# First-layer weights of an attention + MoE kernel split once and kept in DRAM, instead of split again in every quarter

## What is computed

```python
scores = scale * np.matmul(q, k.transpose(0, 1, 3, 2))
kth = np.partition(scores, -32, axis=-1)[..., -32:-31]
scores = np.where(scores >= kth, scores, -1000000000.0)
attn = softmax(scores)            # exp(s - max) / (sum + 1e-9)
x = heads_to_columns(attn @ v)    # 1152 x 512
h = x @ w_in                      # 512 x 2048
x2 = (h * (1.0 / (1.0 + np.exp(-h)))) @ w_out
P = balanced(exp(x2 @ w_gate))    # 1152 x 8
for e in range(8):
    out += P[:, e:e + 1] * (np.maximum(x2 @ w1[e], 0.0) @ w2[e])   # w1: 512 x 1024
```

## Time and profile before

| | |
|---|---|
| median of 3 runs | 1369.2 us (1368.82 to 1369.33) |
| the profiled execution: span from first to last instruction | 1366.2 us |
| between that span and the median | 3.0 us |
| first quarter (attention alone) | to about 118 us |
| quarters with attention and slices | about 118 to 507 us |
| slices alone | about 507 to 562 us |
| experts | from about 562 us |
| TensorE busy | 1350.0 us, 99% |
| VectorE, ScalarE, GpSimd busy | 733.3, 490.3, 351.1 us |
| DMA | 82.16 MB in packets, 18.5% of the engines' time |

### The profile page before, as it was taken

How to read it: one execution, slowest core, us unless ns; L and a number is a source line. 1 busy time by engine, 2 the same in 40 slices (tenths; PEclk the granted TensorE clock), 3 DMA queues, 4 the chain that set the end, 5 groups by cost and what they waited for, 6 DMA issues and landing times.

```text
span 1366.2 us, 21083 instructions
## 1 busy us (share of the span) xinstructions
PE 1350.0 (99%) x8021; PEld 1197.5 (88%) x8021; DVE 733.3 (54%) x1561; ACT 490.3 (36%) x1040; POOL 351.1 (26%) x305
## 2 busy tenths in 40 slices
PE   8999999999999999999999999999999999999999
PEld 6887888788878889989989989989989988998997
DVE  6999989998999975652222222222222222222222
ACT  3446766766675645402112202202211211211210
POOL 0004434534553543212112202202202211211200
PEclk9999999999999999999999999999999999999999
DMA  2033223222231223211011001001101101101001
GB/s 55 23 95 110 89 66 114 84 84 86 90 119 54 93 94 124 93 63 62 19 44 62 31 31 61 31 30 61 61 0 61 61 0 61 61 17 45 0 0 69
DMA packets 59745, 82.16 MB, mean 60 GB/s; under 512 B 17568, under 2 KB 25760, under 8 KB 59680
## 3 DMA queue, kind: packets, MB, share of 16 engines
q1 hardware_dynamic: 59680, 81.30, 18.5%
HBM read 78.92 MB, written 2.36 MB: 59 GB/s over the span
## 4 chain that ended last, share of the span: by engine, by line
PE 94%; DVE 3%; DMA 1%; ACT 1%; issue 1%; POOL 0%; SPq 0%; ACTq 0%
PE banks L322 24%; PE banks L323 24%; PE banks L324 23%; PE banks L377 6%; PE banks L353 5%; PE banks L450 4%; PE banks L361 3%; PE banks L371 2%; PE banks L333 2%; PE banks L336 1%; PE banks L349 1%; DVE rest L747 1%; DVE stats L736 1%; DVE probs L757 1%; PE banks L391 0%
## 5 line engine op out<-in xcount | busy, mean ns | idle before, releaser
L970 POOL TENSOR_TENSOR wu_lo<-wu_raw,wu_hi 128x512 fp32r<-128x512 f32 x116 | 148.7, 1307 | 725.1 <-ACT wu_hi L639 718.3
L696 ACT ACTIVATE h_hi<-banks 128x384 fp32r<-128x384 f32 x192 | 94.5, 492 | 617.4 <-PE banks L324 617.4
L871 DVE SCALAR_TENSOR_TENSOR h_lo<-banks,h_hi 128x384 fp32r<-128x384 f32 x192 | 106.8, 557 | 281.3 <-ACT h_hi L696 281.3
L322 PE MATMUL banks<-x_lo,wu_hi 128*128 128x384 f32 x768 | 257.3, 335 | 0.0
L324 PE MATMUL banks<-x_hi,wu_hi 128*128 128x384 f32 x768 | 256.8, 334 | 0.0
L323 PE MATMUL banks<-x_hi,wu_lo 128*128 128x384 f32 x768 | 256.7, 334 | 0.0
L913 DVE SCALAR_TENSOR_TENSOR y_acc<-banks,plan_e,y_acc 128x512 f32<-128x512 f32 x135 | 101.4, 751 | 265.1 <-PE banks L324 265.1
L323 PE MATMUL banks<-wd_hi,h_lo 128*128 128x512 f32 x576 | 226.8, 394 | 0.0
L322 PE MATMUL banks<-wd_lo,h_hi 128*128 128x512 f32 x576 | 226.0, 392 | 0.0
L324 PE MATMUL banks<-wd_hi,h_hi 128*128 128x512 f32 x576 | 223.7, 388 | 0.0
L970 POOL TENSOR_TENSOR wd_lo<-wd_raw,wd_hi 128x512 fp32r<-128x512 f32 x112 | 144.7, 1313 | 93.7 <-ACT wd_hi L639 93.7
(11 more groups left out here) (100 smaller groups left out, 1979.6 us busy)
## 6 DMA issues: line engine op xcount, KB each, us to landing
wu_raw<-in_moe_w_in_dram SPq DMA_DIRECT2D x16, 1024.0 KB, 5.3
wd_raw<-in_moe_w_out_dram SPq DMA_DIRECT2D x16, 1024.0 KB, 5.4
wu_raw<-in_moe_w_dram SPq DMA_DIRECT2D x16, 1024.0 KB, 5.0
wd_raw<-in_moe_w_dram SPq DMA_DIRECT2D x16, 1024.0 KB, 5.2
k_nat<-in_k_dram SPq DMA_DIRECT2D x32, 128.0 KB, 2.0
v_nat<-in_v_dram SPq DMA_DIRECT2D x32, 128.0 KB, 2.3
q_nat<-in_q_dram SPq DMA_DIRECT2D x32, 72.0 KB, 2.2
out_dram<-y_acc SPq DMA_DIRECT2D x9, 256.0 KB, 2.0
```

The costliest lines, as they stand in the source:

```text
L322: pe.matmul(to, a_hi, b_lo, start=first, stop=False)
L696: act.activation(h_hi[:, f, CH * c:CH * (c + 1)], ps_up[:, at % UBANKS, 0:CH], ACT.Relu).then_inc(h_hi_done, 1)
L871: dve.scalar_tensor_tensor(h_lo[:, f, toks], ps_up[:, at % UBANKS, 0:CH], 0.0, h_hi[:, f, toks].bitcast(F32), ALU.max, ALU.subtract).then_ ...
L970: pool.tensor_tensor(w_lo[stream][:, slot, piece, :], raw[stream][:, piece, :], w_hi[stream][:, slot, piece, :].bitcast(F32), ALU.subtract ...
```

## The change

Each first-layer unit is split once, in steps 1 to 16 of the first quarter, in the order of units 2, 3, 0, 1 (`SPLIT_ORDER`). When a unit's parts are done, SyncE stores both as 1 MB each to a DRAM tensor with 8 KB per partition in a row (`keep_unit`) and only then loads the next raw unit of that stream. Units 0 and 1 stay in the two slots for the first quarter's slices. Every later unit is fetched as two 1 MB transfers straight into `w_hi` and `w_lo` (`fetch_unit`), at the steps of `FETCHES`, once the slot's last user on TensorE is through. TensorE waits for these transfers instead of for the split. The experts' units are split as before; their counts start at 4 instead of 16, and the first of them is split at steps 13 and 16 of the last stage where it was 15 and 17.

```diff
-SPLITS = {2: ("down", 1), 4: ("up", 2), 8: ("up", 3), 9: ("down", 2), 12: ("down", 3), 14: ("up", 4),
-          16: ("up", 5), 17: ("down", 4)}
-LAST_SPLITS = {2: ("down", 1), 4: ("up", 2), 8: ("up", 3), 9: ("down", 2), 12: ("down", 3), 15: ("up", 4),
-               17: ("down", 4)}
+SPLIT_ORDER = (2, 3, 0, 1)
+SPLITS = {1: ("up", 0), 3: ("down", 0), 5: ("up", 1), 7: ("down", 1), 9: ("up", 2), 11: ("down", 2),
+          13: ("up", 3), 15: ("down", 3), ALL + 13: ("up", 4), ALL + 16: ("down", 4)}
+FETCHES = {5: ("up", 2), 7: ("up", 3), 11: ("down", 2), 12: ("down", 3),
+           13: ("up", 4), 15: ("up", 5), 19: ("down", 4), 20: ("down", 5)}
...
+def fetches_at(step):
+    found = []
+    for qr in (step // NT - 1, step // NT - 2):
+        at = step - NT * (qr + 1)
+        if at in FETCHES and 0 <= qr < QUARTERS:
+            stream, u = FETCHES[at]
+            if UQ * qr + u < NU1:
+                found.append((stream, UQ * qr + u))
+    return found
...
+            def keep_unit(stream, n):
+                u = SPLIT_ORDER[n]
+                sp.wait_ge(lo_split[stream], PARTS * (n + 1))
+                for part, parts in zip(kept[stream], (w_hi, w_lo)):
+                    sp.dma_start(part[u], parts[stream][:, u % 2, :, :].bitcast(F32)).then_inc(stored_w[stream][u % 2], 16)
+            def fetch_unit(stream, n):
+                u = n % UQ
+                sp.wait_ge(stored_w[stream][u % 2], 32 if u >= SLOTS else 64)
+                if stream == "up":
+                    sp.wait_ge(up_done, UF * (n - 1))
+                else:
+                    sp.wait_ge(down_done, slices_done(n - 2, KD - 1))
+                for part, parts in zip(kept[stream], (w_hi, w_lo)):
+                    sp.dma_start(parts[stream][:, u % 2, :, :].bitcast(F32), part[u]).then_inc(fetched[stream][u % 2], 16)
...
-            for qr in range(QUARTERS + 1):
-                head(qr, 3)
-                down(qr - 1, 1)
-                up(qr - 1, 2)
-                head(qr, 4)
...
+            load_head(0, 2)
+            load_split("up", 0)
+            load_split("down", 0)
+            for step in STEPS:
+                if step < ALL and TILES[step % NT][1] == 0:
+                    hh = H * (step // NT) + TILES[step % NT][0] + 3
+                    if hh < H * QUARTERS:
+                        load_head(hh // H, hh % H)
+                begun = split_at(step - 3)
+                if begun:
+                    stream, n = begun
+                    if n < UQ:
+                        keep_unit(stream, n)
+                    load_split(stream, n + 1)
+                for stream, n in fetches_at(step):
+                    fetch_unit(stream, n)
...
+            def weights_there(stream, n):
+                if n < SLOTS:
+                    pe.wait_ge(lo_split[stream], PARTS * (SPLIT_ORDER.index(n) + 1))
+                else:
+                    pe.wait_ge(fetched[stream][n % 2], 32 * (n // 2))
...
                     if piece == 0:
                         act.wait_ge(loaded[stream], 16 * (n + 1))
-                        if stream == "up":
-                            need(act, up_done, UF * (n - 1))
-                        elif n >= 2:
-                            act.wait_ge(down_done, slices_done(n - 2, KD - 1))
-                    split_piece(stream, n, n % 2, piece)
+                        if n >= UQ and stream == "up":
+                            act.wait_ge(up_done, UF * (NU1 - 1))
+                        elif n >= UQ:
+                            act.wait_ge(down_done, slices_done(NU1 - 2, KD - 1))
+                        elif n >= SLOTS:
+                            act.wait_ge(stored_w[stream][unit_split(n) % 2], 32)
+                    split_piece(stream, n, unit_split(n) % 2, piece)
```

More of the change, by code:

```diff
@@ L100, in split_at @@
 def split_at(step):
[L102 to L108, removed]
+    return SPLITS.get(step)
 def pieces_at(step, second):
@@ L116, in pieces_at, with unit_split @@
             found.append(begun + (piece,))
+    return found
+def unit_split(n):
+    return SPLIT_ORDER[n] if n < UQ else n - UQ
+def fetches_at(step):
[6 more added lines that the diff above has]
+                found.append((stream, UQ * qr + u))
     return found
@@ L207, in build @@
         lo_split = {"up": sem("wu_lo_split"), "down": sem("wd_lo_split")}
+        stored_w = {s: [sem("kept_" + s + str(i)) for i in range(SLOTS)] for s in ("up", "down")}
+        fetched = {s: [sem("fetched_" + s + str(i)) for i in range(SLOTS)] for s in ("up", "down")}
         up_done, down_done = sem("up_done"), sem("down_done")
@@ L218, in build @@
         raw = {"up": wu_raw, "down": wd_raw}
+        kept = {stream: [nc.dram_tensor("kept_" + stream + "_" + part, (UQ, P, PARTS, UNIT), F32).ap()
+                         for part in ("hi", "lo")] for stream in ("up", "down")}
         w_hi = {"up": wu_hi, "down": wd_hi}
@@ L270, in load_unit @@
                 sp.dma_start(raw[stream][:, :, :], source).then_inc(loaded[stream], 16)
[L272 to L284, removed]
@@ L286, in _ @@
-            head(0, 0)
-            head(0, 1)
-            sp.dma_start(gate_raw[:, :, :], x_gate.rearrange("(a p) e -> p a e", p=P)).then_inc(gate_in, 16)
-            head(0, 2)
-            for qr in range(QUARTERS + 1):
-                head(qr, 3)
-                down(qr - 1, 1)
-                up(qr - 1, 2)
-                head(qr, 4)
[L296 to L307, removed]
@@ L308, in _, with load_split @@
-            down(QUARTERS - 1, 5)
+            def load_split(stream, n):
+                if n < UQ:
+                    load_unit(stream, n, (w_in_u if stream == "up" else w_out_u)[SPLIT_ORDER[n]])
+                else:
+                    load_unit(stream, n, (w1_u if stream == "up" else w2_u)[0, n - UQ])
+            def keep_unit(stream, n):
[3 more added lines that the diff above has]
+                    sp.dma_start(part[u], parts[stream][:, u % 2, :, :].bitcast(F32)).then_inc(stored_w[stream][u % 2], 16)
@@ new lines, in _ @@
+            load_head(0, 0)
+            load_head(0, 1)
+            sp.dma_start(gate_raw[:, :, :], x_gate.rearrange("(a p) e -> p a e", p=P)).then_inc(gate_in, 16)
+            load_head(0, 2)
[9 more added lines that the diff above has]
+                    stream, n = begun
+                    if n < UQ:
+                        keep_unit(stream, n)
+                    load_split(stream, n + 1)
+                for stream, n in fetches_at(step):
+                    fetch_unit(stream, n)
@@ L309, in _ @@
+            load_split("down", UQ + 1)
             with sp.Fori(1, E) as e:
                 for half in range(HALVES):
-                    load_unit("up", NU1 + HALVES * e + half, w1_u[e, half])
-                    load_unit("down", NU1 + HALVES * e + half, w2_u[e, half])
+                    load_unit("up", UQ + HALVES * e + half, w1_u[e, half])
+                    load_unit("down", UQ + HALVES * e + half, w2_u[e, half])
             for t in range(TT):
@@ L409, in silu_slice @@
                     if m == 0:
-                        pe.wait_ge(lo_split["up"], PARTS * (n + 1))
+                        weights_there("up", n)
                         if u == 0:
@@ L423, in silu_slice @@
                     if m == 0:
-                        pe.wait_ge(lo_split["down"], PARTS * (n + 1))
+                        weights_there("down", n)
                         pe.wait_ge(g_lo_done, UF * (n + 1))
@@ L501, in expert_up @@
                 if at == 0:
-                    pe.wait_ge(lo_split["up"], PARTS * (NU1 + he + 1))
+                    pe.wait_ge(lo_split["up"], PARTS * (UQ + he + 1))
                 if isinstance(he, int) and count < UBANKS:
@@ L518, in expert_down @@
                 if t == 0:
-                    pe.wait_ge(lo_split["down"], PARTS * (NU1 + he + 1))
+                    pe.wait_ge(lo_split["down"], PARTS * (UQ + he + 1))
                 if t % (CH // P) == 0:
@@ L705, in expert @@
                     relu(he, at)
-                    n = NU1 + he + 1
+                    n = UQ + he + 1
                     if at == 2 and not last:
@@ L815, in split_pieces @@
                     dve.wait_ge(hi_split[stream], PARTS * n + piece + 1)
-                    dve.tensor_tensor(w_lo[stream][:, n % 2, piece, :], raw[stream][:, piece, :],
-                                      w_hi[stream][:, n % 2, piece, :].bitcast(F32),
+                    dve.tensor_tensor(w_lo[stream][:, unit_split(n) % 2, piece, :], raw[stream][:, piece, :],
+                                      w_hi[stream][:, unit_split(n) % 2, piece, :].bitcast(F32),
                                       ALU.subtract).then_inc(lo_split[stream], 1)
@@ L1000, in _ @@
             pool.partition_all_reduce(top[:, 1:2], top[:, 0:1], P, bass.bass_isa.ReduceOp.max).then_inc(all_max, 1)
-            split("up", NU1 + 1, 1)
-            split("down", NU1 + 1, 1)
+            split("up", UQ + 1, 1)
+            split("down", UQ + 1, 1)
```

(4 more changed lines are left out.)

## The result

The changed kernel takes 1387.4 us (1387.04 to 1388.39, 4 runs) against 1369.0 us in the same session: ratio 1.0137, 95% interval 1.0123 to 1.0152, **18.4 us slower**. Forecast were 1381.4 us (1373 to 1391), slower. The profiled execution has a span of 1385.4 us, 19.2 us above that of before.

What follows compares the result with a forecast made beforehand. The prediction took TensorE to bound the kernel: waits of 4.2 and 9.6 us plus 2.4 for the clock, less 4.0 of relief, gave +12.2 us. Span 1366.2 became 1378.4, plus 3.0 to the median: 1381.4 us, range 1373 to 1391.

Steps and rivals of the forecast that it cites:

- the relief: TensorE's waits on engines that split weights, between 20 and 570 us, shrink: 4.0 us back, bounds 0 and 4.4.
- the three g_f waits: TensorE's waits for g_f: two of 0.4 us after delayed masks, one of 1.3 us in the last stage; all go.
- it starts about 1 us sooner: GpSimd's x_lo subtraction, with two weight pieces gone before it, starts about 1 us sooner, enough for two 0.4 us g_f waits.
- The 0.9 us for pT: TensorE's matmul waits for pT between 20 and 570 us, 0.9 us, counted among the waits on engines that split weights.
- The hidden terms: Fetches in later quarters cost zero; first-quarter collisions of VectorE's masks with GpSimd's pieces cost zero, at most 4 us.
- The two waits: First quarter: ScalarE waits for late raw units, so TensorE waits for pT and loses 4.2 and 9.6 us.
- by a hair: Last two raw units of the first quarter land 0.4 us early and 0.4 us late, against 0.7 us of idle: no loss.
- The clock: TensorE runs slow behind the second first-quarter wait, costing 2.4 us, and not behind the first; bounds 0 and 5.2.
- (a): First quarter: stores don't delay the raw load; first wait covered, second loses 5.4 us; 1373.0 us, chance 0.13.
- (b): First quarter: the queue binds, stores a third slower, three transfers over 11 us, clock 7.6 us in all; 1390.2 us, chance 0.17.
- (c): Faster: first-quarter raw units land before 47 and 59 us, leaving only 4.4 us of gain; 1364.8 us, chance 0.04.
- (d): Nothing measurable: stores don't delay the load, clock stays high, 5.4 us lost against 4.4 gained; 1370.2 us, chance 0.04.

Runs made afterwards that it cites:

- e1: The changed kernel with each unit's two stores and the next raw load one SyncE step earlier, ahead of the head load: 1364.8 us, ratio 0.9969.
- e6: e1 with 4 filler products instead of 6 at the end of each first-quarter step: median 1362.4 us, ratio 0.9951.
- e7: The kernel before the change with 4 filler products instead of 6 at the end of each first-quarter step: 1363.9 us, ratio 0.9970.
- e2: The changed kernel with the next raw load issued ahead of the two stores, at the same places of SyncE's order: 1374.9 us, ratio 1.0048.
- e5: e1 with every part stored a second time, to a DRAM tensor that nothing reads: 1373.5 us, ratio 1.0041.
- e3: The changed kernel with 16 more filler products on TensorE in step 6 and 38 in step 8, in place of its waits: 1382.9 us, ratio 1.0103.

## Why the prediction was right, and where its sizes were off

**What bounds the kernel, and that the relief is small: right.** ScalarE lost 48 us and GpSimd 98 us for a return of some 4 us: e1, which has all of the relief and none of the waits, is 4.3 us below before (2.6 to 5.9 by its interval; the two profiled executions differ by 2.5); the sum over the change's own trace gives 3.2. Forecast 4.0. The work removed was 48 us of ScalarE, not 60, and 98 of GpSimd with 25 of VectorE for 125, which changes nothing at the end. Of the relief's parts, the three g_f waits went. The mask that took 2.67 us at 268.35 us takes 1.35 us in e1, whose x_lo began 1.9 us ahead of it instead of 0.6; so the step "it starts about 1 us sooner" held, but it was not isolated by a run. The 0.9 us for pT at the last turn of quarters I had put down to split pieces: the pieces are gone and the wait is there, in the change and in e1. That step failed. In e1's trace TensorE has nothing between the transposes and the product that needs pT.

**The hidden terms: right.** Fetches cost nothing: no TensorE wait for fetched weights in any trace, and 2.5 us of idle TensorE in the change from 135 to 526 us, where the same work had 3.6. The collisions of masks with GpSimd in the first quarter cost nothing in e1, where masks took up to 1.5 us and TensorE waited for none; with fewer fillers, in e6 and e7, TensorE does wait for VectorE.

**The two waits: right in place, 1.8 us short.** Forecast 4.2 and 9.6 us for TensorE, measured 4.7 and 10.9. The first unit landed at 52.1 us, not 51.1. The second landed 11.9 us behind its first store, not 10.6: SyncE needed 2.16 us to issue the second store (0.43 for the first unit's), so the raw load was issued 2.8 us behind the first store instead of 1.0. (No run isolates this.) That SyncE was free only at 66.0 us (forecast 62.2) did not lengthen the wait: the low clock behind the first wait had moved the time at which ScalarE wants the unit as far, to 65.0 us (forecast 61.25). In steps 9 to 15 TensorE waited for nothing, as forecast. It was as near as the forecast had it, "by a hair": for the unit of step 13, which was to be 0.4 us early, ScalarE waited 0.8 us at 118.45 us.

**The clock: the term that was mis-sized.** Forecast 2.4 us, once; measured 6.8 us, twice. Two things were wrong. The words "none behind the first, which is shorter" took the start's 5 us as a threshold that no row had shown to be one; the clock fell within a wait of 4.7 us. And behind the second the low level lasted 7.6 us of work, not the 4 to 5 us of the start. (That the start is at the low level is read from durations alone: the granted clock stands at 1.00 from 0 to 20 us in the traces of before and after.) The Trainium skill's rule that an idle TensorE falls to the low level, by which I said the first wait might cost as much again, was borne out; the sum by it (1383.8) was nearer. The three errors have one sign: 1.8 for the waits, 4.4 for the clock and 0.8 for the relief (3.2, not 4.0) are the 7.0 us between the forecast +12.2 and the +19.2 of the spans. No error hid another.

**The rivals.** (a) fell: the queue keeps order, and e2 shows what it would have been worth with the load first, 1374.9 us against the 1373.0 worked out. (b) came true in part: three transfers took 11.2 and 11.9 us, over the 11 us that were its sign. But the surplus over 10.6 was 0.6 and 1.3 us instead of 1.8 each, the second with a slow issue in it, and TensorE had no wait at steps 13 and 15. Its 7.6 us for the clock were nearer to the 6.8 measured, so its 1390.2 missed by 2.8 us where the forecast missed by 6.0. e5 shows what a full queue costs. (c) is what e1 is: 1364.8 measured, 1364.8 forecast for that rival. (d) needed the load to overtake the stores as (a) did, and fell with it.

## What to carry to other kernels

Work taken from engines beside the bound returns only the waits that the bound shows, here some 4 us for 146 of ScalarE and GpSimd. When such a change moves transfers, follow each in the issuing queue's program order, past every wait that stands before it: the loss of 18 us came from two loads that stood behind a head's load and two stores, and moving five lines gave it back with profit. Where fillers hold TensorE at speed, give a wait a price for the clock besides its length: behind waits of 4.7 to 11.5 us it was 2.6 to 3.9 us here. Behind shorter ones it ran from nothing to a low clock of 31 us, so removing fillers lowered the median and brought single runs over 12 us longer.

## What was not expected of the hardware

- The clock fell around short waits, and not around every one. It fell with waits of 2.3 us (e5, within the wait), 1.4 us (e6, 0.1 us behind its end), 1.9 us (e3, 1.5 us behind) and 1.1 us (e5, 1.8 us behind). It held with waits of 1.7 us (e6 and e7) and 1.0 us (e2). In e6 it stayed low for 31 us, of which TensorE was busy 30.2; the same kernel kept 0.998 to 1.000 in its other runs. Up to 143.15 us this was work of transposes, small products and fillers; then the first feed-forward products began, and at 146.6 us the clock was high again. What decides when it falls and how long it stays low is open. The Trainium skill ("TensorE: Matmul & The Clock Gate", "What's actually happening") says that activity releases the throttle; here work of transposes, small products and fillers did not for 27 us.
- Issuing a DMA on SyncE took 2.16 us instead of 0.3 to 0.9 when the same queue already held a head's loads and a 1 MB store. Stores and 8 KB rows are not needed for it: in e1 small loads of heads took up to 1.4 us each to issue behind 1 MB transfers (and one store 1.5), in e5 one took 5.6 us, and the kernel before, without any store of weights, has one of 1.8 us, for q_nat at 122.95 us. What sets it is open.
- Stores of 1 MB land as loads do: kept_down_hi in a median of 4.3 us, kept_up_hi 5.2, the raw units of the first layer, third in line, 10.5 and 9.6 us.
